# Attention head 0 of a three-block kernel: its operands made in place from a second load

## The reference, cut to what matters

```python
q_bits = (np.einsum('bhsd,dk->bhsk', q, proj) > 0)      # k_bits alike
q_bucket = np.sum(q_bits * 2 ** np.arange(6), axis=-1)  # k_bucket alike
mask = q_bucket[:, :, :, None] == k_bucket[:, :, None, :]
scores = np.where(mask, scale * np.matmul(q, k.transpose(0, 1, 3, 2)), -1000000000.0)
attn = softmax(scores)                                  # written out, + 1e-09 in the sum
x = np.matmul(attn, v)          # (2, 768, 512) after the heads are laid side by side
u = x + np.real(fft(fft(x, axis=1), axis=2)); x = u + relu(norm(u) @ w_ch1) @ w_ch2
theta = x @ w_theta; y = w_tok_r @ (x * cos(theta)) + w_tok_i @ (x * sin(theta))
u = x + y; out = u + relu(u @ w_ch)
```

## Time and profile before

| what | us |
|---|---|
| median of 3 runs (738.51 to 738.86) | 738.67 |
| the profiled execution | 738.64 |
| its span, first to last instruction | 736.8 |
| PE busy | 712.6 (97%) |
| DVE, ACT, POOL busy | 410.8, 340.2, 322.7 |

### The profile page before, as it was taken

One profiled execution on the slowest core, in us unless ns is written; L12 is line 12 of the kernel. 1 busy time (PEld: TensorE's weight loads), 2 busy tenths in 40 slices (PEclk: granted clock), 3 DMA queues, 4 the chain that ended last, 5 costly groups with the idle time before them and its releaser, 6 DMA issues.

```text
span 736.8 us, 10909 instructions
## 1 busy us (share of the span) xinstructions
PE 712.6 (97%) x3754; PEld 604.0 (82%) x3754; DVE 410.8 (56%) x827; ACT 340.2 (46%) x689; POOL 322.7 (44%) x283
## 2 busy tenths in 40 slices
PE   3999999999999999999999999999999999999998
PEld 2788898889888877888888888888888888888876
DVE  2998899889989587833131122211343556845443
ACT  1899999999999644333101111111233334223101
POOL 3798888878888257955100000020034555121100
PEclk9999999999999999999999999999999999999999
DMA  6464753333332012522000001020011220000002
GB/s 167 115 158 116 179 133 95 104 104 97 95 80 55 1 44 87 152 69 80 1 0 1 1 0 43 2 78 1 1 43 44 86 56 24 1 28 16 15 28 86
DMA packets 39400, 45.77 MB, mean 62 GB/s; under 512 B 15796, under 2 KB 26676, under 8 KB 39348
## 3 DMA queue, kind: packets, MB, share of 16 engines
q1 hardware_dynamic: 36564, 41.65, 20.6%
q0 software_dynamic: 2784, 3.43, 1.8%
HBM read 28.16 MB, written 3.15 MB: 42 GB/s over the span
## 4 chain that ended last, share of the span: by engine, by line
PE 79%; DVE 12%; issue 4%; ACT 2%; DMA 1%; POOL 1%; SPq 1%; ACTq 0%; POOLq 0%; DVEq 0%
PE PS L890 21%; PE PS L892 21%; PE PS L891 21%; DVE negmax L1235 5%; DVE ETL L1244 3%; PE PS L981 3%; PE PS L1021 3%; PE PS L1006 2%; PE PS L1007 2%; PE PS L1022 2%; PE PS L1109 1%; DVE bias L1237 1%; ACT E L775 1%; ACT OS L787 1%; PE PS L992 1%
## 5 line engine op out<-in xcount | busy, mean ns | idle before, releaser
L1387 DVE SCALAR_TENSOR_TENSOR HL<-PS,HH 128x512 fp32r<-128x512 f32 x48 | 33.2, 691 | 154.6 <-ACT HH L876 154.6
L876 ACT ACTIVATE HH<-PS 128x512 fp32r<-128x512 f32 x48 | 28.7, 598 | 181.4 <-PE PS L892 181.4
L1235 DVE TENSOR_REDUCE negmax<-PS 128x1 f32<-128x768 f32 x96 | 91.0, 948 | 28.0 <-PE PS L1007 27.9
L775 ACT ACTIVATE E<-PS,bias,factor 128x768 f32<-128x768 f32 x96 | 95.5, 995 | 21.6 <-DVE factor L1238 15.0
L1244 DVE TENSOR_TENSOR ETL<-PS,ETH 128x384 fp32r<-128x384 f32 x192 | 97.2, 548 | 2.8 <-ACT ETH L768 2.8
L768 ACT ACTIVATE ETH<-PS 128x384 fp32r<-128x384 f32 x192 | 83.1, 485 | 8.2 <-PE PS L981 8.0
L981 PE MATMUL PS<-ident,E 128*128 128x128 f32 x576 | 79.7, 273 | 0.1
L1021 PE MATMUL PS<-ETH,VHL 128*128 128x384 f32 x192 | 72.4, 377 | 4.7 <-ACT OS L787 4.7
L1006 PE MATMUL PS<-TOPH,TOPL 128*128 128x512 f32 x192 | 69.1, 360 | 7.2 <-DMA KM<-MR 6.2
L890 PE MATMUL PS<-UTH,W 128*128 128x512 f32 x192 | 75.8, 395 | 0.2 <-issue 0.2
L892 PE MATMUL PS<-UTH,W 128*128 128x512 f32 x192 | 74.8, 390 | 0.0
(11 more groups left out here) (173 smaller groups left out, 1562.3 us busy)
## 6 DMA issues: line engine op xcount, KB each, us to landing
RAW<-in_moe_w_ch_dram SPq DMA_DIRECT2D x32, 256.0 KB, 2.8
QK<-in_qk_dram SPq DMA_DIRECT2D x16, 384.0 KB, 4.2
QM<-TOPH SPq DMA_DIRECT2D x16, 192.0 KB, 2.9
KM<-TOPL SPq DMA_DIRECT2D x16, 192.0 KB, 3.2
VR<-in_v_dram SPq DMA_DIRECT2D x16, 192.0 KB, 2.7
TOPL<-QM SPq DMA_DIRECT2D x16, 192.0 KB, 2.7
TOPH<-TOPH SPq DMA_DIRECT2D x16, 192.0 KB, 3.0
out_dram<-fin SPq DMA_DIRECT2D x12, 256.0 KB, 2.0
```

The lines of the kernel that those rows point to most:

```text
L775: nc.scalar.activation(E[:, tile % NE, :], s_bank(tile)[:, 0:S], ACT.Exp, bias=bias[:, t:t + 1], scale=factor[:, t:t + 1], accum_out=esum[ ...
L1235: nc.vector.tensor_reduce(negmax[:, t:t + 1], s_bank(tile)[:, 0:S], AX_X, ALU.max, negate=True).then_inc(s_max, 1)
```

## The change

Head 0 no longer goes through the split, the moves and the bits units that the other heads use:

- The host appends a seventeenth "head" to `qk`: k of head 0 in rows 0 to 63 and q in rows 64 to 127. SP loads it into the third buffer of `E` right behind the plain load. With q and k each present in both halves, ACT writes q high to `QM` and to the lower half of `TOPL` and k high to the lower half of `TOPH`, POOL writes k high to the upper half of `TOPH` and k low to `KM`, DVE writes q low to the upper half of `TOPL`. No DMA moves a piece of head 0.
- Projection, signs and thresholds are packed into one table `const`, issued from ACT's queue. POOL makes the signed projection and its parts.
- Head 0's bits are two plain float32 matmuls of the unsplit `QK` (512 and 256 columns) into a score bank, and DVE compares into `QM` and `KM` directly. The key side starts at row 32 of the 44 columns (`KROW`, `MW`), for all heads.
- Head 1 is split by ACT and DVE, as head 0 was.
- TensorE multiplies zeros (a piece of `E` that DVE clears): two float32 matmuls of 384 columns at the start, two of 128 behind the bits.
- On SP's queue the load of QK of head 2 now waits for head 0's operands; semaphore counts are shifted by one head.

```diff
--- before.py
+++ after.py
...
 NM = 2 * BITS
+KROW = 32
+MW = KROW + NM
 SCALE = D ** -0.5
...
 
-    slots = [(None, None, None, [("bits", 0, i) for i in range(2)])]
+    slots = [(None, None, None, [])]
     for n in range(NH * QT):
...
     einv = put("einv", [P, NSTAT])
-    sign = put("sign", [P, 2 * NM])
-    proj2 = put("proj2", [P, 2 * NM])
-    projH = put("projH", [P, 2 * NM], F32R)
-    projL = put("projL", [P, 2 * NM], F32R)
-    gamma = put("gamma", [2 * NM, 2])
+    const = put("const", [P, 2 * MW + 2])
+    proj2 = put("proj2", [P, MW])
+    projH = put("projH", [P, MW], F32R)
+    projL = put("projL", [P, MW], F32R)
+    gamma = const[0:MW, 2 * MW:2 * MW + 2]
     stats = put("stats", [P, NT, 6])
...
                 b, r = h % 2, h % 3
-                sp.wait_ge(s_top, 2 * (h + 1))
+                sp.wait_ge(s_top, 2 * h)
                 if h >= 2:
...
                 sp.wait_ge(s_ring, done["bits", h, 1])
-                sp.wait_ge(s_away, 32 * (h + 1))
+                sp.wait_ge(s_away, 32 * h)
                 sp.dma_start(TOPL[D:P, r].bitcast(F32), QM[0:D, b].bitcast(F32)).then_inc(s_in, 16)
                 sp.dma_start(TOPH[0:D, r].bitcast(F32), TOPH[D:P, r].bitcast(F32)).then_inc(s_in, 16)
 
             def move_mask(h):
                 b = h % 2
-                if h:
-                    sp.wait_ge(s_mr, h)
-                else:
-                    sp.wait_ge(emptied["bits"], 2)
+                sp.wait_ge(s_mr, h)
                 sp.dma_start(QM[D:D + NM, b].bitcast(F32), MR[0:NM].bitcast(F32)).then_inc(s_mask, 16)
-                sp.dma_start(KM[D:D + NM, b].bitcast(F32), MR[NM:2 * NM].bitcast(F32)).then_inc(s_mask, 16)
+                sp.dma_start(KM[D:D + NM, b].bitcast(F32), MR[KROW:MW].bitcast(F32)).then_inc(s_mask, 16)
 
             load_qk(0)
-            sp.dma_start(proj2[:], projb).then_inc(s_const, 16)
-            sp.dma_start(sign[:], sign_in).then_inc(s_const, 16)
-            sp.dma_start(gamma[:], gamma_in).then_inc(s_const, 16)
+            sp.dma_start(E[:, NE - 1, :], qk[NH]).then_inc(s_turned, 16)
             load_qk(1)
+            load_v(0)
             sp.dma_start(ident[:], ident_in).then_inc(s_ident, 16)
-            move_away(0)
-            load_v(0)
-            move_in(0)
-            move_mask(0)
             load_qk(2)
...
                 b, r = h % 2, h % 3
-                pool.wait_ge(s_sq, h)
-                pool.wait_ge(s_top, 2 * h)
+                pool.wait_ge(s_sq, h - 1)
+                pool.wait_ge(s_top, 2 * (h - 1))
                 if h >= 3:
                     pool.wait_ge(s_s, QT * (h - 2))
                 nc.gpsimd.tensor_copy(TOPH[:, r], QK[:, b]).then_inc(s_top, 1)
-                pool.wait_ge(s_top, 2 * h + 1)
+                pool.wait_ge(s_top, 2 * h - 1)
                 nc.gpsimd.tensor_tensor(TOPL[:, r], QK[:, b], TOPH[:, r].bitcast(F32), ALU.subtract).then_inc(s_top, 1)
 
             def mask_rows(h):
-                pool.wait_ge(emptied["bits"], 2 * (h + 1))
-                pool.wait_ge(s_mask, 32 * h)
+                pool.wait_ge(emptied["bits"], 2 * h)
+                if h >= 2:
+                    pool.wait_ge(s_mask, 32 * (h - 1))
                 nc.gpsimd.tensor_scalar(MR[:], MB[:], gamma[:, 0:1], gamma[:, 1:2], ALU.is_gt, ALU.mult).then_inc(s_mr, 1)
...
             early = [(dst, src, s_table) for dst, src in tables]
-            scale_q(1)
+            turned = E[:, NE - 1, :]
+            pool.wait_ge(s_init, 4)
+            pool.wait_ge(s_const, 16)
+            nc.gpsimd.tensor_tensor(proj2[:], const[:, 0:MW], const[:, MW:2 * MW], ALU.mult).then_inc(s_proj, 1)
+            pool.wait_ge(s_proj, 1)
+            nc.gpsimd.tensor_copy(projH[:], proj2[:]).then_inc(s_proj, 1)
+            pool.wait_ge(s_proj, 2)
+            nc.gpsimd.tensor_tensor(projL[:], proj2[:], projH[:].bitcast(F32), ALU.subtract).then_inc(s_proj, 1)
+            pool.wait_ge(s_proj, 3)
+            pool.wait_ge(s_turned, 16)
+            nc.gpsimd.tensor_copy(TOPH[0:D, 0], turned[0:D]).then_inc(s_first_key, 1)
+            pool.wait_ge(s_first_key, 1)
+            nc.gpsimd.tensor_tensor(KM[0:D, 0], turned[0:D], TOPH[0:D, 0].bitcast(F32), ALU.subtract).then_inc(s_first_key, 1)
+            pool.wait_ge(s_first_key, 2)
+            pool.wait_ge(s_top, 2)
+            split_v(0)
             for slot, (tile, et, pv, us) in enumerate(slots):
                 h, t = divmod(slot - 1, QT)
                 if slot and t == 0:
-                    if h == 0:
-                        split_top(1)
-                        split_v(0)
-                    elif h > 1:
+                    if h > 1:
                         finish(h - 2, 1)
...
 
+            act.dma_start(const[:], const_in).then_inc(s_const, 16)
             act.wait_ge(s_qk[0], 16)
+            nc.scalar.activation(QM[0:D, 0], QK[0:D, 0], ACT.Copy, scale=SCALE).then_inc(s_first_high, 1)
+            act.wait_ge(s_turned, 16)
+            nc.scalar.activation(TOPL[D:P, 0], E[D:P, NE - 1, :], ACT.Copy, scale=SCALE).then_inc(s_first_high, 1)
+            nc.scalar.activation(TOPH[D:P, 0], QK[D:P, 0], ACT.Copy).then_inc(s_first_high, 1)
+            act.wait_ge(s_qk[1], 16)
             act.wait_ge(s_init, 2)
-            nc.scalar.activation(TOPH[:, 0], QK[:, 0], ACT.Copy, scale=qscale[:]).then_inc(s_top, 1)
+            nc.scalar.activation(TOPH[:, 1], QK[:, 1], ACT.Copy, scale=qscale[:]).then_inc(s_top, 1)
             for slot, (tile, et, pv, us) in enumerate(slots):
...
                             act.wait_ge(s_mr, h - 1)
-                        nc.scalar.activation(MB[:, c], ring(unit_no[u])[0:2 * NM, 0:HC], ACT.Copy).then_inc(emptied["bits"], 1)
+                        nc.scalar.activation(MB[:, c], ring(unit_no[u])[0:MW, 0:HC], ACT.Copy).then_inc(emptied["bits"], 1)
                     elif kind == "back":
...
                     c = slice(i * HC, (i + 1) * HC)
-                    pe.wait_ge(s_top, 2 * (h + 1))
-                    if h == 0 and i == 0:
+                    pe.wait_ge(s_top, 2 * h)
+                    if h == 1 and i == 0:
                         pe.wait_ge(s_proj, 3)
-                    last = product(bank[0:2 * NM, 0:HC], projH[:], TOPH[:, h % 3, c], projL[:], TOPL[:, h % 3, c], True, True)
+                    last = product(bank[0:MW, 0:HC], projH[:], TOPH[:, h % 3, c], projL[:], TOPL[:, h % 3, c], True, True)
                 elif kind == "back":
                     pe.wait_ge(emptied["pv"], 2 * h + i + 1)
                     for j in range(HALF):
                         last = nc.tensor.transpose(bank[:, j * P:(j + 1) * P], OS[:, i, j * P:(j + 1) * P], ident[:])
                 last.then_inc(s_ring, 1)
 
+            blank = E[:, 0, 0:HC]
+            pe.wait_ge(s_blank, 1)
+            for _ in range(2):
+                nc.tensor.matmul(OT, blank[:, 0:P], blank, start=True, stop=True)
+            pe.wait_ge(s_proj, 1)
+            pe.wait_ge(s_qk[0], 16)
+            nc.tensor.matmul(s_bank(1)[0:MW, 0:512], proj2[:], QK[:, 0, 0:512], start=True, stop=True)
+            nc.tensor.matmul(s_bank(1)[0:MW, 512:S], proj2[:], QK[:, 0, 512:S], start=True, stop=True).then_inc(s_first_bits, 1)
+            for _ in range(2):
+                nc.tensor.matmul(OT[:, 0:P], blank[:, 0:P], blank[:, 0:P], start=True, stop=True)
+
             for tile, et, pv, us in slots:
                 if tile is not None:
                     h, t = divmod(tile, QT)
-                    pe.wait_ge(s_away, 32 * (h + 1))
-                    pe.wait_ge(s_in, 32 * (h + 1))
-                    pe.wait_ge(s_mask, 32 * (h + 1))
+                    if tile == 0:
+                        pe.wait_ge(s_first_high, 3)
+                        pe.wait_ge(s_first_key, 2)
+                        pe.wait_ge(s_first_low, 1)
+                        pe.wait_ge(s_first_mask, 2)
+                    elif t == 0:
+                        pe.wait_ge(s_away, 32 * h)
+                        pe.wait_ge(s_in, 32 * h)
+                        pe.wait_ge(s_mask, 32 * h)
                     if tile >= 2:
...
 
-            dve.wait_ge(s_const, 16 * 3)
-            nc.vector.tensor_tensor(proj2[:], proj2[:], sign[:], ALU.mult).then_inc(s_proj, 1)
-            dve.wait_ge(s_proj, 1)
-            nc.vector.tensor_copy(projH[:], proj2[:]).then_inc(s_proj, 1)
-            dve.wait_ge(s_proj, 2)
-            nc.vector.tensor_tensor(projL[:], proj2[:], projH[:].bitcast(F32), ALU.subtract).then_inc(s_proj, 1)
+            nc.vector.memset(E[:, 0, 0:HC], 0.0).then_inc(s_blank, 1)
+            dve.wait_ge(s_first_high, 1)
+            nc.vector.scalar_tensor_tensor(out=TOPL[0:D, 0], in0=QK[0:D, 0], scalar=SCALE, in1=QM[0:D, 0].bitcast(F32),
+                                           op0=ALU.mult, op1=ALU.subtract).then_inc(s_first_low, 1)
+            dve.wait_ge(s_const, 16)
+            dve.wait_ge(s_first_bits, 1)
```

(55 more changed lines are left out.)

## The result

| | before | after |
|---|---|---|
| median of the runs, us | 738.76 (4 runs, 738.51 to 738.87) | 734.25 (4 runs, 732.72 to 734.83) |
| ratio of the times | 1 | 0.9934, 95% interval 0.9922 to 0.9945 |
| profiled execution, us | 738.64 | 734.04 |
| its span | 736.8 | 731.4 |
| time less span, all runs | 1.75 to 1.85 | 2.52 to 2.93 |

The kernel is faster by 0.7%, 4.5 us, against 7.1 forecast (731.6). The median, 734.25, stands outside the likeliest case's own range (730.8 to 732.3) and 0.25 us above the end of the stated one (730.6 to 734.0); as a ratio to the kernel before, 0.9934 lies just inside it (734.0 of 738.64 is 0.9937).

A forecast was written before the change was run, and what follows sets the result against it. PE was taken to run nearly gapless from tile 6 on, so only the start-up before it could shrink. From 738.64 us, -5.8 for tile 0's earlier start and -1.2 for the fill gave 731.6, range 730.6 to 734.0.

The forecast's parts named there:

- the likeliest case: Whole kernel: tile 0 early and the clock up in the fill, 731.6 us, own range 730.8 to 732.3, chance 55%.
- The bound and the carry: From tile 6 on, PE has nearly no gap, so a shift of that tile shifts the end; 709.4 us unchanged.
- The moves: Start of head 0: two moves away, two moves in and two mask DMAs leave the chain (5.9 to 14.1).
- T = 8.4: Start of tile 0's scores, set by bits and DVE's two comparisons: 8.4 us instead of 14.24, a term of -5.8.
- POOL's path: POOL's cast and subtraction for head 0 after the second load: ready at 8.1 us (7.6 to 9.0), contention 0.05.
- The fill, -1.2: From tile 0 to tile 6: PE at the upper clock level shortens the 13.1 us by 1.2; at the lower, 0.
- the rival with 20%: Clock down again at tile 0's start after PE's idling: the fill stays 13.1 us, time 732.8; chance 20%.
- another case, T at 9.6 with the clock down: Tile 0's scores start late, at about 9.6 us, and the clock is down too: 734.0 us; chance 4%.
- The hand-over: Head 1's moves before tile 6: some 0.5 us of slack stays; rival, 2 us later gives 733.1, chance 4%.

The follow-up runs named there:

- e7_move_dma: Changed kernel without the second load: ACT and DVE split 128 rows and four DMAs move head 0's halves; measured 738.43 us.
- e3_nozero: Changed kernel without its four zero products; measured 734.76 us.
- e8_best: Changed kernel with three 384-column zero products behind the bits, table first on SP's queue, head 0's QK on ACT's, projection on DVE; 732.62 us.
- f3_short: As e8_best, with zero products of 384 and 256 columns ahead of the bits and two of 384 behind instead of three; measured 732.76 us.
- e2: Changed kernel with three zero products of 384 columns behind head 0's bits instead of two of 128; measured 732.47 us.
- e5: Kernel before the change with zero products alone added, three at the start and nine before tile 0's scores; measured 737.48 us.
- e1_const_sp: Changed kernel with the packed table issued from SP's queue between head 0's two loads instead of ACT's; measured 733.69 us.

## Why the prediction was right, and where it was not

- **The bound and the carry.** Right. From tile 6 to DVE's last addition there are 706.98 us before and 706.92 after. The shift of tile 6, 27.35 to 21.93, is 5.4 us, and the span shrank by 5.4 (736.8 to 731.4).
- **The moves.** Right: they leave the chain, and e7_move_dma shows that the second load is what does it.
- **T = 8.4.** Measured 8.85, on the path named, DVE's masks behind the bits. Its terms: the table came last, not QK (it landed at 3.9, then POOL worked until 4.32), so bits started at 4.37 and not 3.9; they took 2.05 (1.9 forecast), the comparisons 1.07 each (1.1). I had the table's landing at 3.0 from a small DMA that was issued late; one issued from ACT's queue beside the first large load took 3.2 to 3.4 us, in four traces. The Trainium skill's four passes (FP8 and Floating Point Precision, TensorE Precision Notes) agree with the trace: 256 columns at the upper level took 0.45 us, 4.2 times the 0.107 of one pass over 256 columns at 2.4 GHz, and 0.87 at the lower. The bits came out near 1.9 only because the clock rose during them, while in e3_nozero they took 2.8; that this term was nearly met is luck.
- **POOL's path.** 8.1 forecast, 8.45 measured, and the weighing of the Trainium skill's rule failed. The second load was there at 4.9, earlier than the 5.3 forecast, but POOL was held in its subtraction for the projection until 5.69. I read 1.80 against 1.85 as contention of 0.05, but DVE's work beside the 1.85 read PSUM and one SBUF tile. Where DVE read two SBUF tiles (4.60 to 5.55), POOL's subtraction of 44 columns took 1.01, though a multiply of the same size had taken 0.28, and in e8_best the cast took 1.43 instead of 0.82, beside DVE's 4.95 to 5.90. In e7_move_dma the same subtraction began 0.03 before DVE's and took 0.28:

```profile
5.02 0.28 POOL L660 TENSOR_TENSOR projL<-proj,projH 128x44 fp32r<-128x44 f32 x1
```

  It is as if POOL had stood while DVE ran, but only where DVE began first. It cost nothing in the changed kernel, since DVE's masks end later, and became the bound in f3_short.
- **The fill, -1.2.** This step failed: "what an idle time of 2 does is not in the trace. I say yes" was the text's answer on whether the clock holds. PE stood from 7.0 to 8.85 with two short zero products ahead, and the scores of tiles 0 and 1 ran at 0.50, so L stayed 13.08. The size was right: bridged, L is 11.76 in the changed kernel (e2) and 11.80 in the kernel before (e5), and the second exponential of e2 begins 3.7 after T (12.82), as the forecast had it. This is the rival with 20%. The one execution of the changed kernel with 732.72 has a span of 730.2, that of the bridged kernel, at a recorded clock of 1.000, so it seems to have kept the clock; it was not traced.
- **Outside the span, 0.** The prediction does not name this term, and so puts it at nothing without a reason. Time less span grew from 1.8 to a median of 2.7, and why is open. The sum closes with it: 731.6, + 0.45 of T, + 1.2 of the fill, + 0.8 outside = 734.05, against 734.04 for the profiled execution. The range's upper end, 734.0, stood for another case, T at 9.6 with the clock down; that the measured time lies so near to it is chance.
- **The hand-over** held: tile 6 waited for no DMA in the changed kernel, nor in e2 with its shorter fill.

## What to carry to other kernels

A start-up made of serial DMA rounds between on-chip tiles can be replaced by loading the same data twice in the layouts wanted: each round here was about 3 us, and the second load landed 1.2 after the first. Filling TensorE's waits with zero products pays in full only if they come near enough to the first real product: here a rest of 0.3 to 1.2 us kept the clock, and one of 1.8 lost it in both traces that have it. They must not outrun the data either; size them at both clock levels. When judging contention between POOL and DVE, look for a row in which DVE reads two SBUF operands; one with a PSUM operand says nothing.

## What the runs showed of the hardware

- PE idle for 1.8 us (7.0 to 8.85) was followed by a granted clock of 0.50 from 9 to 12 us; with PE's gap cut to 0.3 us it was 1.00 there in e2_bridge, and 512 columns took 0.23 us instead of 0.43. Gaps of 1.0 us (f3_short) and 1.2 us (e5_before_zeros) kept the upper level too. After the gap of 1.8 us in e1_const_sp the first products of tile 0 were still at the upper level, and the granted clock was 0.50 from 11 to 13 us. Mean clock and span differ between executions of one kernel (0.998 with 731.4 to 731.9 us, and 1.000 with 730.2).
- The clock record can miss the lower level at a kernel's first work: in the kernel before it says 1.00 while 384 columns take 0.32 us, which is 1.2 GHz; in e3_nozero it says 1.00 while 512 columns take 0.43 us (10.53 in its chain).
- Operations of POOL that begin while one of DVE's with two SBUF operands runs are stretched: 0.28 to 1.01 for 44 columns, 0.82 to 1.43 for 768. The Trainium skill (GPSIMD Engine Reference, Specifications) states this contention; by that rule, the trace agrees.
- Two executions of one program can differ outside the span by 1 us (e7_move_dma: 1.98 to 2.98), while the kernel before keeps to 0.1.
